# The last two down tiles of an expert's step, multiplied bank by bank

## The reference

```python
h = x @ w_in
g = h * (1.0 / (1.0 + np.exp(-h)))
x = (g @ w_out)
...
for e in range(E):
    h = np.maximum(x @ w1[e], 0.0)
    ye = h @ w2[e]
    out += P[:, e:e + 1] * ye
```

## Time and profile before

| | |
|---|---|
| median of 3 runs | 1346.96 us (1346.21 to 1347.03) |
| the profiled execution | 1346.58 us, of it the span from first to last instruction 1344.8 us |
| mean granted TensorE clock | 0.999 |
| TensorE busy | 1326.9 us, 99% of the span |
| VectorE, ScalarE, GpSimd busy | 799.6, 610.0, 317.7 us |

### The profile page before, as it was taken

The page is one execution under the profiler, slowest core; times in us unless marked ns, Lnnn a source line. Parts: engine busy times, 40 slices in busy tenths (PEclk is TensorE's granted clock), DMA queues, the critical chain, the costliest instruction groups (busy, mean ns, idle before and its releaser), DMA issues.

```text
span 1344.8 us, 20944 instructions
## 1 busy us (share of the span) xinstructions
PE 1326.9 (99%) x7884; PEld 1216.7 (90%) x7884; DVE 799.6 (59%) x1461; ACT 610.0 (45%) x1300; POOL 317.7 (24%) x370
## 2 busy tenths in 40 slices
PE   7999999999999999999999999999999999999998
PEld 6889999999889898989989898989898998989896
DVE  8878486667685464646464557646464646545452
ACT  7865264444534262625353444526252534435250
POOL 6543122403031313032130403130312304040200
PEclk9999999999999999999999999999999999999999
DMA  9722212312122212222221212321221212121112
GB/s 331 233 89 86 64 63 64 95 34 87 38 70 73 79 48 79 70 72 78 59 88 42 95 40 86 95 78 50 90 80 53 76 62 95 32 95 48 63 32 64
DMA packets 53000, 106.67 MB, mean 79 GB/s; under 512 B 5793, under 2 KB 15009, under 8 KB 52897
## 3 DMA queue, kind: packets, MB, share of 16 engines
q1 hardware_dynamic: 52896, 105.29, 24.5%
HBM read 102.12 MB, written 3.15 MB: 78 GB/s over the span
## 4 chain that ended last, share of the span: by engine, by line
PE 91%; DVE 6%; ACT 1%; issue 1%; POOL 0%; DVEq 0%; POOLq 0%; ACTq 0%
PE bank L731 39%; PE bank L666 39%; PE bank L728 10%; PE bank L585 1%; PE bank L568 1%; DVE hid_l L1360 1%; PE bank L552 1%; DVE hid_h L1358 1%; DVE up_l L1310 1%; ACT parts L983 1%; ACT prob L849 1%; DVE parts L1340 0%; DVE parts L1345 0%; PE bank L594 0%; DVE prob L1195 0%
## 5 line engine op out<-in xcount | busy, mean ns | idle before, releaser
L666 PE MATMUL bank<-xc_h,up_h 128*128 128x384 f32 x1120 | 376.0, 336 | 2.4 <-ACT bank L972 1.5
L666 PE MATMUL bank<-xc_h,up_l 128*128 128x384 f32 x1120 | 375.0, 335 | 0.0
L666 PE MATMUL bank<-xc_l,up_h 128*128 128x384 f32 x1120 | 374.9, 335 | 0.0
L731 PE MATMUL bank<-down_h,hid_l 128*128 128x512 f32 x768 | 299.7, 390 | 0.0
L731 PE MATMUL bank<-down_l,hid_h 128*128 128x512 f32 x768 | 299.6, 390 | 0.0
L731 PE MATMUL bank<-down_h,hid_h 128*128 128x512 f32 x768 | 299.4, 390 | 0.0
L478 POOL TENSOR_TENSOR up_raw<-up_raw 128x256 f32<-128x256 f32 x80 | 71.3, 892 | 905.6 <-DMA up_raw<-w_up 905.6
L1310 DVE TENSOR_TENSOR up_l<-up_raw,up_h 128x512 fp32r<-128x512 f32 (+1 forms) x234 | 200.4, 889 | 51.6 <-ACT up_h L910 50.3
L666 PEld LDWEIGHTS bank<-xc_h,up_h 128*128 128x128 f32 x1120 | 210.2, 188 | 8.0 <-issue 2.9
L666 PEld LDWEIGHTS bank<-xc_l,up_h 128*128 128x128 f32 x1120 | 210.2, 188 | 2.7
L666 PEld LDWEIGHTS bank<-xc_h,up_l 128*128 128x128 f32 x1120 | 210.2, 188 | 0.0
(11 more groups left out here) (126 smaller groups left out, 1438.6 us busy)
## 6 DMA issues: line engine op xcount, KB each, us to landing
up_raw<-w_up SPq DMA_DIRECT2D x80, 512.0 KB, 3.5
down_raw<-w_down SPq DMA_DIRECT2D x160, 256.0 KB, 2.7
v_sb<-vw SPq DMA_DIRECT2D x44, 256.0 KB, 4.3
k_sb<-kw SPq DMA_DIRECT2D x12, 288.0 KB, 6.1
q_sb<-qT SPq DMA_DIRECT2D x12, 256.0 KB, 5.3
out<-x_sb SPq DMA_DIRECT2D x12, 256.0 KB, 2.6
nraw<-sizes SPq DMA_DIRECT2D x1, 2.0 KB, 2.8
gate_sb<-w_gate SPq DMA_DIRECT2D x1, 16.0 KB, 8.6
```

The lines of the kernel that those rows point to most:

```text
L666: mm = nc.tensor.matmul(ps[:, 0:HALF], a[quad % UP_BUFS][:, w, k, :], b[x][:, k, :], start=(n == 0 and not add), stop=(n == 5), skip_group ...
L731: mm = nc.tensor.matmul(ps[:], x[a][:, t // 3, t % 3 * P:t % 3 * P + P], w[b], start=start, stop=stop)
```

## The change

`down` gets an inner function `feed(j, t)`, the work of one tile on one bank, and `next_step(t)`, which places P1 and P5 of the next step. Where the step is an expert's and not GATE (steps 5 to 19), tiles 6 and 7 are now done bank by bank: bank 0 gets its three matmuls of tile 6 and its three of tile 7, then bank 1, and so on. The waits for `down_ready` and `hid_ready` now stand in `feed`, so that they are made again for every bank, in all steps. P1 and P5 stand behind banks 3 and 4 as before, each now six matmuls apart.

```diff
--- before.py
+++ after.py
@@ -710,36 +710,47 @@
                     bank_free = [(hid_ready, 4 * quad2 + 1), (summed, 2 * quad2 + 1), (summed, 2 * quad2 + 2),
                                  (hid_ready, 4 * quad3 + 1), (summed, 2 * quad3 + 1), (summed, 2 * quad3 + 2),
                                  (hid_ready, 4 * quad3 + 1), (hid_ready, 4 * quad3 + 4)]
-                    for j in range(FT):
-                        f = down_order[j]
-                        tile = s * FT + j
+                    def feed(j, t):
+                        f, tile, ps = down_order[j], s * FT + j, banks[t]
                         pe.wait_ge(down_ready, tile + 1)
                         pe.wait_ge(hid_ready, 4 * (s * FP + f % FP) + (2 if f < FP else 4))
                         w = (down_h[:, tile % DOWN_BUFS, :], down_l[:, tile % DOWN_BUFS, :])
                         x = (hid_h[:, f, :, :], hid_l[:, f, :, :])
-                        for t, ps in enumerate(banks):
-                            if j == 0:
-                                if t == 3:
-                                    p4(quad3)
-                                pe.wait_ge(*bank_free[t])
-                            for n, (a, b) in enumerate(((0, 0), (0, 1), (1, 0))):
-                                start, stop = j == 0 and n == 0, j == FT - 1 and n == 2
-                                if transposed:
-                                    mm = nc.tensor.matmul(ps[:, 0:HALF], w[a][:, t // 2 * P:t // 2 * P + P], x[b][:, t % 2, :],
-                                                          start=start, stop=stop)
-                                else:
-                                    mm = nc.tensor.matmul(ps[:], x[a][:, t // 3, t % 3 * P:t % 3 * P + P], w[b],
-                                                          start=start, stop=stop)
+                        if j == 0:
+                            if t == 3:
+                                p4(quad3)
+                            pe.wait_ge(*bank_free[t])
+                        for n, (a, b) in enumerate(((0, 0), (0, 1), (1, 0))):
+                            start, stop = j == 0 and n == 0, j == FT - 1 and n == 2
+                            if transposed:
+                                mm = nc.tensor.matmul(ps[:, 0:HALF], w[a][:, t // 2 * P:t // 2 * P + P], x[b][:, t % 2, :],
+                                                      start=start, stop=stop)
+                            else:
+                                mm = nc.tensor.matmul(ps[:], x[a][:, t // 3, t % 3 * P:t % 3 * P + P], w[b],
+                                                      start=start, stop=stop)
+                        if j == FT - 1:
+                            mm.then_inc(down_done, 1)
+                        elif t == len(banks) - 1:
+                            mm.then_inc(down_used, 1)
+
+                    def next_step(t):
+                        if s + 1 < STEPS and t == len(banks) - 3:
+                            p1(s + 1, 0)
+                        if s + 1 < STEPS and t == len(banks) - 2:
+                            p5(s + 1, 0)
+
+                    by_bank = 2 if blocks[s][1] >= HALVES and s != GATE else 0
+                    for j in range(FT - by_bank):
+                        for t in range(len(banks)):
+                            feed(j, t)
                             if j == FT - 1:
-                                mm.then_inc(down_done, 1)
-                                if s + 1 < STEPS and t == len(banks) - 3:
-                                    p1(s + 1, 0)
-                                if s + 1 < STEPS and t == len(banks) - 2:
-                                    p5(s + 1, 0)
-                            elif t == len(banks) - 1:
-                                mm.then_inc(down_used, 1)
+                                next_step(t)
                         if j in after_tile:
                             after_tile[j]()
+                    for t in range(len(banks) if by_bank else 0):
+                        for j in range(FT - by_bank, FT):
+                            feed(j, t)
+                        next_step(t)
 
                 def logits():
```

## The result

| | before | changed |
|---|---|---|
| median of 20 runs each | 1346.45 us (1345.04 to 1347.03) | 1348.50 us (1347.38 to 1350.73) |
| ratio to before | | 1.0016, 95% interval 1.0010 to 1.0022 |
| the profiled execution | 1346.58 us, span 1344.8 | 1350.73 us, span 1349.0 |

The change costs about 2.1 us, within the 0.2% that was called no change, and inside the range. The scatter is wider: before, all runs lie within 2.0 us; now they reach over 3.4 us. The profiled execution is the slowest of the twenty and lies 4.15 us above that of before. Both the usual cost and the scatter have to be explained.

A forecast was written before the change was run, and what follows sets the result against it. TensorE was taken as the bound, waiting for nothing from step 5 on except at the end. Terms 2.1 + 0.3 + 0 - 1.5 = +0.9 us gave 1347.5; allowing for the runs' median, it said 1347.7 us, range 1346.0 to 1349.6.

The forecast's parts named there:

- Tile 7 is wanted earlier: Step 11: tile 7 is wanted 3.40 us earlier, 1.90 us before its split ends; with 0.2 for the restart, +2.1 us.
- The wait lowers the clock: Rival, step 11: TensorE's idle 2.1 us drops the clock to 1.2 GHz, making 1350 to 1356 us; chance 0.03.
- Longer stretches between the shapes: Steps 5 to 18: banks 4 and 5 each get a second triple at 0.69 us instead of 0.68; +0.3 us.
- P1, P5 and P6 keep their neighbours: Steps 5 to 18: the claim that these products stand beside the same work, so only the triples' spacing changes.
- More waits: All steps: 864 added waits hide behind running matmuls; taken as 0, with bounds 0 and 44 us.
- named in a rival: Rival: the added waits cost something, with three per triple in dense tile 0; 1356 us at 10 ns each; chance 0.04.
- The end: Step 19: banks complete every 1.36 us, so stores don't pile up; -2.1 to -0.9 us, taken as -1.5.
- The signs that it named: Changed profile: one `down_l` wait near 836 us, clock 1.00 after 838, one step of 64 us, matmuls 0.227 us apart around waits.

The follow-up runs named there:

- e4: The kernel before with tiles 6 and 7 bank by bank in step 11 alone, waits once per tile: 1348.65 us, ratio 1.0016.
- e7: e5 with the split of tile 7 in step 11 moved ahead of the third quad's up tiles on ScalarE and VectorE: 1345.57 us, ratio 0.9991.
- e5: The changed kernel with each down tile's two waits made once, at bank 0: 1347.73 us, ratio 1.0010.
- e8: e4 with three tiles (5, 6 and 7) bank by bank in step 11 instead of two: 1354.08 us, ratio 1.0056.
- e10: e7 with the two waits repeated for every bank in steps 4 to 19 alone (640 more): 1345.57 us, ratio 0.9993.
- e9: e7 with the two waits repeated for every bank in steps 0 to 3 alone (224 more): 1346.17 us, ratio 0.9998.
- e2: The changed kernel without bank by bank in step 11, repeated waits kept: 1346.74 us, ratio 0.9998.
- e6: The changed kernel without bank by bank in step 11 and with the waits once per tile: 1345.58 us, ratio 0.9993.
- e1: The kernel before, in its order, with the two waits made again for every bank (864 more): 1347.71 us, ratio 1.0005.
- e3: The kernel before with tiles 6 and 7 bank by bank in the last step alone, waits once per tile: 1346.27 us, ratio 0.9998.

## Why the prediction was right or wrong

It was right in its range and in its sign; the sum, +0.9 us, was less than half of the +2.05 measured, and three of the changed kernel's twenty runs lie above the range. That the median fell into the range owes something to luck: the term for the shapes was 0.5 us too high, those for the waits and the end 0.9 and 0.5 us too low, so the errors cancel in part.

*Tile 7 is wanted earlier: +2.1 us.* Right in place and size. e4 shows 2.09 us with this edit alone, e7 shows that it goes with an earlier split. The split ended at the time that was read from the trace of before, and the allowance of 0.2 us for the restart was right (2.16 - 0.23 = 1.93 between the starts, the rest behind it, where the next start comes after 0.34 us and not 0.23).

*The wait lowers the clock: a rival at 0.03.* This chance was set too low. "In the trace the longest waits left the clock where it was" was read from one stretch, with 1.5 us idle; the wait forecast was longer. The changed kernel and e5 show the clock at 1.2 GHz behind it, e4 at full clock behind the same wait: it comes and goes from one execution to the next and costs 1.6 us when it comes. By the mean clocks it came in at least two and at most six of the changed kernel's twenty runs; in e5 three runs of eleven stand in the upper group. So it was worth 0.2 to 0.5 us in the mean, and the median, whose runs are at 1.000, has none of it. The rival's price, 2 to 8 us of work at the low clock, stood in no row; it was a bit over 3 us. The other rule that was cited, an idle array drops to half rate (the Trainium skill, TensorE: Matmul & The Clock Gate, section "Part 1: The HAM clock gate"), agrees with e8, the changed kernel and e5, and not with e4's profile, where the clock stayed at 1.00.

*Longer stretches between the shapes: +0.3 us.* Wrong in sign. The second triples do start 0.69 us apart, 1.39 for two. But P5, and with it P6, lost some of its own irregular spacing: 1.04 us behind six matmuls of 512 columns and not 1.06. "P1, P5 and P6 keep their neighbours" was the step that failed. A step is 61.96 instead of 61.97 us, 13 ns less before rounding, so the term is about -0.2.

*More waits: 0.* Right for the experts' steps (e10), where the matmuls behind the waits start 0.23 us apart. Wrong for the dense steps, which the prediction named in a rival and then priced from a row where nothing holds the sequencer up. The last line of the earlier trace rows, which it counted under down tiles, is one for the hidden values `hid_l`: each dense step has this place, the last bank of tile 0. There the weight load is held back until VectorE is done, even where TensorE's matmuls go on without a gap. In step 2, the kernel before, then the changed one (PEld is TensorE's weight load):

```profile
246.84 0.55 DVE L1360 TENSOR_TENSOR hid_l<-parts,hid_h 128x384 fp32r<-128x384 f32 x1
247.44 0.19 PEld L728 LDWEIGHTS bank<-hid_h,down_h 128*128 128x128 f32 x1
```

```profile
248.36 0.56 DVE L1371 TENSOR_TENSOR hid_l<-parts,hid_h 128x384 fp32r<-128x384 f32 x1
249.03 0.19 PEld L726 LDWEIGHTS bank<-hid_h,down_h 128*128 128x128 f32 x1 [0.20 <-issue]
```

From VectorE's end to the weight load it is 0.05 us before (247.39 to 247.44) and 0.11 with the change (248.92 to 249.03). A wait instruction of 51 ns now stands between the two, and nothing covers it: the bank starts 0.24 us behind its forerunner (248.82 to 249.06) and not 0.17 (247.29 to 247.47). That happens once in each dense step and makes some 0.3 us. The other part, 0.4 to 0.7 us in one dense step of an execution, goes with a longer cast on VectorE: one or both of the two casts to `hid_h` in front take 0.57 us or more and not 0.46 and 0.36. It stood in all four profiles with waits repeated in the dense steps, and in one (e5) of the eight others. In e10's step 0 it is the other way round: a cast that takes 0.82 us in all other profiles takes 0.36. Together: 0.6 to 1.2 us by e9 against e10, e2 against e6, e1 against before, and e5 against the changed kernel. Each single one of these is near what the runs can tell; all four go the same way. Whether the waits shift VectorE and GpSimd against each other, or the long casts and the waits fall together by chance, stays open.

*The end: -1.5 us.* Right in mechanism, too large: -1.0, next to the smaller of its bounds. The stores no longer pile up, but the last one still takes 3.4, 3.5 and 3.6 us (the changed kernel, e3, e7) and not 2.4, and in all three an instruction load on q8 stands in the same stretch. No run is without that load, so that it is the cause is likely and not shown. The Trainium skill, DMA: Bandwidth & Descriptors, section "Why a DMA increments its semaphore by 16 and not by 1", has the engines finish independently and the semaphore count them all; from that the prediction drew that the slowest engine sets this term, nearer to -0.9, and the -1.0 of the profiles agrees.

*The signs that it named.* The wait for `down_l`, the stores and the takes came as described. The clock after 838 us did not stay at 1.00 in the profiled execution, so its long step is 65.67 us and not 64, and in the dense steps matmuls behind added waits do start over 0.23 us apart, which by its own words makes it wrong there.

Put together from the measured sizes: 2.1 - 0.2 - 1.0 + 0.9 for the waits = +1.8 us, and 1.6 more where the clock falls. The runs' median is at +2.05. The scatter is the clock's in part; e1, which has only the waits, also reaches over 2.4 us, at mean clocks of 0.999 and 1.000.

## What to carry to other kernels

When an engine without slack will consume something earlier, list the time at which every such input is ready in every step, not in a typical one: fourteen of fifteen steps had 7 us to spare, and the one with other work in front made as much loss as the whole change. Price a new wait on TensorE with what the idle time may do to its clock. And leave repeated waits out of inner loops where the engine's next instruction is held up by another wait, since there each one is on the path.

## What the runs showed of the hardware

The same idle time of 1.78 us left the clock at 1.00 in one execution (e4) and was followed by 0.50 in others (the changed kernel, e5); the matmuls of 512 columns then start 0.43 us apart instead of 0.23, for a bit over 3 us. After 5.12 us idle the clock was at 0.50 before work began again (e8); that was so in the one execution that was profiled, and the mean clock of 0.997 says the same of the other four.

A wait instruction of 51 ns that is already fulfilled costs nothing while matmuls run, at 0.17 us apart and at 0.23 (e10; in e1 a step stays at 61.97 us). It costs about 0.07 us where the next weight load is being held back for another engine: there the distance is 0.24 to 0.25 us and not 0.17.

A product of six 128x384 matmuls takes 1.06 us behind three matmuls of 128x512 (P5 before) and behind a long run of them (P1), and 1.04 behind six (P5 in the changed kernel). So a change of shape has no fixed price. Why six cost less than both three and many, no run here shows.
